# Who stores x and who splits the first expert's weights, in an attention kernel with two mixtures behind it

## Time and profile before

| | us |
|---|---|
| median of 3 runs | 774.54 (773.97 to 779.65) |
| profiled execution | 770.29, span 768.4 |
| TensorE busy | 671.6 (87%) |
| VectorE, ScalarE, GpSimd busy | 371.6, 316.2, 198.1 |
| x of the last tile written from | 114.80 |
| first product of an expert | 151.10 |

### The profile page before, as it was taken

One profiled execution on the slowest core, in us unless ns is written; L12 is line 12 of the kernel. 1 busy time (PEld: TensorE's weight loads), 2 busy tenths in 40 slices (PEclk: granted clock), 3 DMA queues, 4 the chain that ended last, 5 costly groups with the idle time before them and its releaser, 6 DMA issues.

```text
span 768.4 us, 13788 instructions
## 1 busy us (share of the span) xinstructions
PE 671.6 (87%) x3958; PEld 553.7 (72%) x3958; DVE 371.6 (48%) x649; ACT 316.2 (41%) x509; POOL 198.1 (26%) x252
## 2 busy tenths in 40 slices
PE   5778884599999999999999999959669998999894
PEld 4566763387878878878788787849547876778673
DVE  2655867544444436254353454411736656456621
ACT  2376962144444344244343444411024655455511
POOL 1527603412222222222312222200312222222321
PEclk9799997799999999999999999965579999999998
DMA  9998829255646445456254464636126657667211
GB/s 191 217 222 229 226 64 339 90 161 124 182 130 175 127 96 154 92 140 161 69 152 122 111 191 122 184 104 202 45 82 191 216 174 261 191 196 244 43 41 15
DMA packets 91086, 116.66 MB, mean 152 GB/s; under 512 B 52260, under 2 KB 52388, under 8 KB 90976
## 3 DMA queue, kind: packets, MB, share of 16 engines
q1 hardware_dynamic: 77664, 94.19, 41.1%
q0 software_dynamic: 9568, 21.37, 14.7%
q10 hardware_dynamic: 3808, 0.56, 0.5%
HBM read 99.72 MB, written 20.71 MB: 157 GB/s over the span
## 4 chain that ended last, share of the span: by engine, by line
PE 77%; DVE 6%; SPq 6%; issue 3%; DMA 3%; ACT 2%; POOLq 0%; POOL 0%; ACTq 0%; DVEq 0%
PE bank L683 61%; PE bank L699 5%; SPq L410 4%; PE bank L614 3%; PE bank L658 3%; DVE col_val L1176 3%; PE bank L763 1%; PE bank L603 1%; DMA x_att<-x_sb 1%; SPq L425 1%; DVE w_lo L1085 1%; SPq L417 1%; PE bank L575 1%; ACT w_hi L796 1%; PE bank L533 1%
## 5 line engine op out<-in xcount | busy, mean ns | idle before, releaser
L1085 DVE TENSOR_TENSOR w_lo<-stage,w_hi (+1 forms) x128 | 152.4, 1224 | 29.3 <-ACT w_hi L796 26.6
L683 PE MATMUL bank<-w_hi,xt_hi 128*128 128x512 f32 x336 | 140.0, 417 | 16.0 <-DVE w_lo L1085 7.9
L1232 DVE TENSOR_TENSOR ht_lo<-bank,ht_hi 128x512 fp32r<-128x512 f32 x84 | 58.1, 691 | 183.5 <-ACT ht_hi L882 183.5
L796 ACT CAST w_hi<-stage (+1 forms) x128 | 129.1, 1049 | 25.5 <-PEq L725 23.0
L683 PE MATMUL bank<-w_hi,ht_hi 128*128 128x512 f32 x336 | 138.8, 413 | 0.0
L683 PE MATMUL bank<-w_lo,xt_hi 128*128 128x512 f32 x336 | 134.4, 400 | 0.0
L683 PE MATMUL bank<-w_lo,ht_hi 128*128 128x512 f32 x336 | 131.2, 391 | 0.0
L879 ACT ACTIVATE h_sb<-bank 128x512 f32<-128x512 f32 x84 | 50.3, 599 | 112.6 <-PE bank L683 111.8
L683 PE MATMUL bank<-w_hi,xt_lo 128*128 128x512 f32 x336 | 92.6, 398 | 0.0
L683 PE MATMUL bank<-w_hi,ht_lo 128*128 128x512 f32 x336 | 91.1, 392 | 0.0
L882 ACT CAST ht_hi<-bank 128x512 fp32r<-128x512 f32 x84 | 49.3, 587 | 100.6 <-PE bank L699 100.6
(11 more groups left out here) (112 smaller groups left out, 727.7 us busy)
## 6 DMA issues: line engine op xcount, KB each, us to landing
stage<-in_moe_w SPq DMA_DIRECT2D x128, 512.0 KB, 3.6
v_win<-in_v SPq DMA_DIRECT2D x24, 192.0 KB, 4.7
x_moe<-zeros SPq DMA_DIRECT2D x13, 256.0 KB, 3.0
x_att<-x_sb SPq DMA_DIRECT2D x12, 256.0 KB, 4.1
x_sb<-x_moe SPq DMA_DIRECT2D x12, 256.0 KB, 2.7
out<-x_moe SPq DMA_DIRECT2D x4, 768.0 KB, 8.5
late_raw<-in_v SPq DMA_DIRECT2D x6, 384.0 KB, 6.6
stage<-in_k SPq DMA_DIRECT2D x6, 256.0 KB, 7.0
```

What stands on the lines that cost most here:

```text
L683: last = eng.matmul(ps[:], *every[i], start=(i == 0), stop=(i == len(every) - 1))
L796: eng.copy(piece(w_hi[n % SETS], j), stage[:, j, :]).then_inc(s_hi, 1)
L1085: eng.tensor_tensor(piece(w_lo[n % SETS], j), stage[:, j, :], piece(w_hi[n % SETS], j).bitcast(F32), ALU.subtract)\
L1232: eng.tensor_tensor(ht_lo[:, half].rearrange("p k n -> p (k n)"), ps_ht[half][:], ht_hi[:, half].bitcast(F32).rearrange("p k n -> p (k n)" ...
```

## The change

- POOL issues the stores of x: that of tile t after window 2t+7, those of the last three tiles between its new splits.
- POOL rounds and splits the first expert's weights itself, a copy and a subtraction for each piece, after its loop over the windows and before `lanes(0)`. ScalarE and VectorE no longer do it within the steps.
- SP loads windows 4 and 5 ahead of k of batch 1; q of batch 1 in thirds after the windows of tiles 0, 2 and 3; the values of batch 1 at tile 1. The first expert's pieces are loaded at tiles 4 to 7 instead of 2 to 5, with up to two in flight. SP issues no store of x.
- All q jobs are copied out by VectorE, where it did so only at steps -1 and 2.
- TensorE makes the router's logits of tiles 10 and 11 after the last step.

```diff
-        ON_DVE, ON_DVE_AT = "q", (-1, 2)
+        ON_DVE = "q"
...
-        FIRST_SPLIT = 14
-        PIECE_TILE = 2
+        PIECE_TILE = 4
...
+                elif n == 1:
+                    eng.wait_ge(s_first, j + 1)
                 else:
-                    eng.wait_ge(s_lo, g - PIECES + 1)
+                    eng.wait_ge(s_lo, g - 2 * PIECES + 1)
...
-            for j in range(JOBS):
-                load_tiles("k", 1, j)
             for w in range(4, WR):
                 load_window(w)
             for j in range(JOBS):
-                load_tiles("q", 1, j)
-            for hh in range(2):
-                load_values(1, hh)
+                load_tiles("k", 1, j)
             for t in range(NT):
                 for w in (2 * t + WR, 2 * t + WR + 1):
                     if w < BATCH * NWIN:
                         load_window(w)
-                land(0)
+                if t in (0, 2, 3):
+                    load_tiles("q", 1, max(t - 1, 0))
+                if t == 1:
+                    for hh in range(2):
+                        load_values(1, hh)
                 if PIECE_TILE <= t < PIECE_TILE + PIECES // 2:
                     for g in range(2 * (t - PIECE_TILE), 2 * (t - PIECE_TILE + 1)):
                         load_piece(g)
-                eng.wait_ge(s_x, t + 1)
-                eng.dma_start(x_dram[t * P:(t + 1) * P, :], x_sb[:, t % 2]).then_inc(s_xst[t % 2], 16)
+                    land(2)
...
-                    eng.wait_ge(s_x, t + 1)
+                    eng.wait_ge(s_x, t + 1 if t < NT - 2 else NT)
...
-                if (t := tile_at(s, GATE_LAG)) is not None:
+                if (t := tile_at(s, GATE_LAG)) is not None and t < NT - 2:
...
+            for t in (NT - 2, NT - 1):
+                wait_job(eng, ("x", t))
+                router_logits(0, t, wgate1, 2 * E)
...
+            def store_x(t):
+                eng.wait_ge(s_x, t + 1)
+                eng.dma_start(x_dram[t * P:(t + 1) * P, :], x_sb[:, t % 2]).then_inc(s_xst[t % 2], 16)
+
+            def split_first(j):
+                eng.wait_ge(s_loaded, j + 1)
+                eng.tensor_copy(piece(w_hi[0], j), stage[:, j, :]).then_inc(s_fhi, 1)
+                eng.wait_ge(s_fhi, j + 1)
+                eng.tensor_tensor(piece(w_lo[0], j), stage[:, j, :],
+                                  piece(w_hi[0], j).bitcast(F32), ALU.subtract).then_inc(s_first, 1)
...
+                if w >= WR and w % 2:
+                    store_x((w - WR) // 2)
+
+            eng.wait_ge(s_tr, job_at["q", 1, 1, JOBS - 1] + 1)
+            split_first(0)
+            store_x(NT - 3)
+            for j in (1, 2):
+                split_first(j)
+            store_x(NT - 2)
+            for j in (3, 4):
+                split_first(j)
+            store_x(NT - 1)
+            for j in range(5, PIECES):
+                split_first(j)
```

More of the change, by code:

```diff
@@ L295, in build @@
         s_loaded = sem("s_loaded")
+        s_first = sem("s_first")
+        s_fhi = sem("s_fhi")
         s_hi = sem("s_hi")
@@ L667, in mixture @@
                     hi, lo = w_hi[n % SETS], w_lo[n % SETS]
-                    eng.wait_ge(s_lo, PIECES * (n + 1))
+                    if n == 0:
+                        eng.wait_ge(s_first, PIECES)
+                    else:
+                        eng.wait_ge(s_lo, PIECES * n)
                     eng.reg_mov(done, 0)
@@ L817, in _ @@
                 for job in at_step.get(s, []):
-                    if not (s in ON_DVE_AT and job[0] in ON_DVE):
+                    if job[0] not in ON_DVE:
                         empty_job(eng, job, eng.copy)
[L820 to L826, removed]
             eng.wait_ge(s_gt[0], NT)
@@ L1082, in split_piece @@
             def split_piece(n, j):
-                eng.wait_ge(s_hi, j + (n * PIECES + 1))
+                eng.wait_ge(s_hi, j + ((n - 1) * PIECES + 1))
                 eng.tensor_tensor(piece(w_lo[n % SETS], j), stage[:, j, :],
@@ L1265, in _ @@
                 for job in at_step.get(s, []):
-                    if s in ON_DVE_AT and job[0] in ON_DVE:
+                    if job[0] in ON_DVE:
                         empty_job(eng, job, eng.tensor_copy)
@@ L1271, in _ @@
                     value_sum(*DVE_SUMS[s])
-                if 0 <= s - FIRST_SPLIT - 1 < PIECES:
-                    split_piece(0, s - FIRST_SPLIT - 1)
             eng.wait_ge(s_router, 16 * 5)
```

## The result

The changed kernel took 783.49 us (median of 18 runs, 778.81 to 786.19) against 775.28 (18 runs, 771.6 to 780.14): ratio 1.0096, interval 1.0074 to 1.0118. That is +8.2 us, where 5.9 were forecast; the interval reaches to both sides of 1%. The profiled execution took 783.36 us with a span of 781.5.

The account below looks back on a forecast made before the run. The experts' products, 61% of the span, bound the kernel and stay untouched; only work before them counts. Attention gains and stalls, then POOL's splits, move the route's end from 143.0 to 148.9: +5.9, 780.5 us, range 774.8 to 792.

Parts of the forecast that it names:

- main step: Before the routing's lanes: POOL's eight pieces at 3.4 us, 27.2 in all, delay the lanes' start to 132.1 from 126.89.
- Tile 2 without its wait: Attention, tile 2: the store of tile 0 on POOL lands in time, so the 4.0 us stall goes; written about 53.8.
- q of batch 1 late: Attention, before tile 4: last third of q lands at 67.7, wanted at 64.8; new TensorE stall of 2.9 us.
- Store 3: Attention, before tile 5: POOL issues this x store at 78.0, landing 82.1; tile 5 stalls 2.25 us (0 to 6).
- Stores 5 and 6 at no margin: Attention, tiles 7 and 8: these x stores land at about 91.6 and 97.7, some 1 us early; no stall.
- rival (2): Attention: POOL's stores gate the tiles, landing in 6.5 us beside weight loads, not 4.1; +5 us, 786; chance 0.12.
- Rival (1): POOL's splits: rounding is slower than a plain copy; at 1 us more per piece +14, 788.5; chance 0.28.
- rival (4): POOL's splits: pieces take 2.3 us and are not the bound; -1.5, or -6.5 without the new stalls; chance 0.04.
- VectorE beside POOL: Routing: six two-tensor VectorE operations meet POOL's pieces; 6.5 us spare, so 1 us for POOL's part (0 to 4).
- Last logits: Attention's last two tiles: router logits moved after the last step; heads 0.55 earlier, +0.4 behind; net about -0.2 us.
- Lanes: Routing, behind POOL's splits: lanes start at 133.1 and end at 147.4, route ends at 148.9 against 143.0.
- Rival (3): Attention: the two new stalls (late q, tile 5's store) don't come; +0.8 us, 775.3; chance 0.14.

Follow-up runs that it names:

- both edits of 3: Changed kernel with the last two thirds of batch 1's q loaded one tile earlier and first expert's weights handled as before the change: 774.87 us, ratio 0.9989.
- Experiment 4: Changed kernel with x stored by SP again, right behind each tile's windows: 776.69 us, ratio 1.0017.
- experiment 6: Changed kernel with x stored by SP, late q one tile earlier, only five pieces split on POOL, three by ScalarE and VectorE: 768.51 us, ratio 0.9905.
- 5: Changed kernel with x stored by SP and the last two thirds of q loaded one tile earlier, all eight splits on POOL: 771.79 us, ratio 0.9967.
- experiment 8: Kernel with five POOL splits, SP stores and earlier q, but q copies of steps 4, 9, 10, 11 by ScalarE: 769.59 us, ratio 0.9916.
- pool0: Changed kernel with x stored by SP, q one tile earlier, first expert's weights handled as before the change: 767.92 us, ratio 0.9913.

## Why the prediction held, point by point

**The sign and the main step were right; that the number fits is partly luck.** Forecast +5.9 (780.5), measured +8.2, within the range of 774.8 to 792 and at the edge between "same" (0.56) and "slower by over 1%" (0.42). The main step, eight pieces on POOL at 3.4 us each in front of the lanes, came as forecast. But the working was done on the profile of before, and from profile to profile the route ends 11.6 later (154.6 against 143.0), twice the 5.9. What failed lies ahead of POOL's chain: it began 4.85 later than forecast (first rounding at 105.45, not 100.6).

- *Tile 2 without its wait*: forecast 53.8, came 53.86. *Tile 3*: 62.3, came 62.73.
- *q of batch 1 late*: data forecast at 67.7 (its terms as written, 61.75 + 0.9 + 0.9 + 4.5, make 68.05), the job began at 68.07. The step that failed is the next one, "tile 4 comes 5.5 after that: 73.2". It came 8.5 after, at 76.61, because TensorE ran at half its clock for the whole stretch 70 to 80. The profile of before had shown it at a smaller size: after the 4.0 us wait of tile 2 four transpositions took 1.08 at 61.2, and the pace was back at 63.74. I had costed a wait at its length only; the size that it had here, up to 83.0, could not be read from that row.
- *Store 3*: forecast issued 78.0 and landing 4.1 later; it was issued at 82.67, since the v jobs ran late and slow, and landed 3.3 later. Tile 5 waited 0.49, not 2.25, and came at 86.01, not 82.1; with q early it waited 2.35, with both edits of 3 4.14, so the wait was real and only hidden by the slow stretch.
- *Stores 5 and 6 at no margin*: tile 8 waited 1.36 for store 6, whose landing took 6.6 us beside two pieces of weights. That is a part of rival (2): POOL's stores landed in 4.8 in the median, SP's before in 4.1. Experiment 4's 6.8 us are more than the forecast's terms, but TensorE's clock is in them; what its profile puts down to the stores is 4.9.
- *POOL's piece*: forecast 3.4, measured 1.05 + 2.36, 3.42 from start to start. Rival (1), a slower rounding, is out; rival (4) too. *Issue of a store*: forecast 1.1, measured 0.55; the indirect DMA was a poor neighbour.
- *VectorE beside POOL*: I took 1 us. The stretch from `score` to the lanes grew by 7.4 us, of which VectorE's spare time hid all but 2.1. With the splits over before it, 6.95 again (experiment 6), with them partly over, 9.3 and 11.3 (5 and 4). I had counted the six two-tensor operations only, but a cast and a tensor_scalar with one input were held as well (0.95 and 1.98). By the rule of the Trainium skill, SBUF — State Buffer, Who interferes with whom, the sum would have been 2 to 4 us higher, an estimate. The trace agrees in kind, since operations lasted until POOL's subtraction ended, and less in size: the lanes were 2.1 later than POOL's end, 1.1 more than the sum had. The row of before (1.50 instead of 1.22) understated it, because there VectorE met short copies.
- *Last logits*: forecast -0.2; tile 11 came 4.40 after tile 10 instead of 4.91, and `score` 5.13 after tile 11 in both kernels: -0.5. That edit leaves TensorE with less to do in the tail, where the clock fell in several of the kernels; whether it has a part in that is not tested, since no run takes it back.
- *q copies on VectorE*: +0.4 at tile 1 as forecast, nothing in all (experiment 8).
- *Lanes*: forecast 133.1, came 138.27, 5.2 later. POOL's chain began 4.85 late, was 0.8 shorter than forecast from its first rounding to its end, and VectorE's part was 1.1 larger. In the profiles the first product is 11.75 later, in the medians the whole is 8.2 longer. The clock has a part in this. The profiled execution of before had a mean granted clock of 0.932. Of the 70 timed ones beside the experiments, those with 0.928 or more took 771.6 to 774.1 us, and those with 0.915 or less 774.8 to 781.2; the changed kernel's profile, with 0.918, is in the middle of its own (0.907 to 0.926). So a fast execution of before was set against a usual one of the changed kernel. Where in the execution the clock differed, the times don't show.

Rival (3), no new stalls, is out by the trace. What the change did was to pay for a 4 us stall with two others and a chain in front of the routing; its parts are not bad in themselves: SP's new order, with q one tile earlier and the stores still on SP, is 0.3% faster than the kernel before with all splits on POOL, 1.0% with five and 0.9% with none. In pool0, the last of these, tile 2 comes 5.2 earlier than before; SP's order, the q copies and the last logits are all in it, and no run takes the order or the logits back alone.

## What to carry to other kernels

Before a transfer or a piece of work is put into another engine's program, list what stands ahead of it there and what waits behind it: here a store inherited two value sums and a wait for scores, and the routing inherited eight splits. Moving work to an idle engine pays only as far as it ends before the chain that also needs that engine, so move part of it. Cost a wait on TensorE at more than its length, and as a range: the slow stretch behind it was none in one trace here and some 15 us in another. Take several executions before a difference of a few us is given to an edit, and look at what runs on VectorE beside a long GpSimd operation.

## What was not expected of the hardware

- After a wait of 3.86 us TensorE's granted clock was 0.50, the lower of its two levels (1.2 GHz), from 70 to 80, though it was 9.76 us busy in them; 28 idle transpositions in front of the last 2.1 us of the wait did not prevent it (0.52).
- The same wait of 2.11 us was followed by groups at half pace in one profile and at full pace in another (twelve transpositions 2.82 and 1.53).
- A VectorE operation on 12 elements per partition lasted 1.98 us beside a GpSimd subtraction, and a cast with a single input took 0.95 instead of 0.19.
- GpSimd rounds 128x1024 to fp32r in 1.05 us, as fast as ScalarE (1.05), and is busy only 0.55 us with a plain store of 256 KB, half of an indirect one of the same size (1.09).
